# Moving one scatter of the last chunk behind the fetch of the first tile's second rows

## The reference

```python
# 1. linear attention with decay, B=4, H=8, S=768, head_dim 48
y[:, :, t] = einsum('bhd,bhde->bhe', rt, state + (u * kt) outer vt)
state = w * state + kt outer vt
x = y as (3072, 384)
# 2. mixture of experts, top 1 of E=8, F=1024, with a skip
do_compute = x @ w_skip > 0
e_idx, gate_w = argmax and top softmax probability of x @ w_gate
x[i] += gate_w * (relu(x[i] @ w1[e]) @ w2[e])      # rows with do_compute
# 3. dense layer, d_ff 2048
h = x @ w_in;  out = (h * clip(h + 3, 0, 6) / 6) @ w_out
```

## Time and profile before

| | us |
|---|---|
| median of 3 runs | 697.08 (696.63 to 697.37) |
| profiled execution, its own time | 699.52 |
| its span in the profile | 697.7 |
| PE busy | 686.7 (98%) |
| DVE busy | 381.7 (55%) |
| ACT busy | 323.8 (46%) |
| POOL busy | 141.2 (20%) |

### The profile page before, as it was taken

One profiled execution on the slowest core, in us unless ns is written; L12 is line 12 of the kernel. 1 busy time (PEld: TensorE's weight loads), 2 busy tenths in 40 slices (PEclk: granted clock), 3 DMA queues, 4 the chain that ended last, 5 costly groups with the idle time before them and its releaser, 6 DMA issues.

```text
span 697.7 us, 13712 instructions
## 1 busy us (share of the span) xinstructions
PE 686.7 (98%) x5072; PEld 623.7 (89%) x5072; DVE 381.7 (55%) x788; ACT 323.8 (46%) x704; POOL 141.2 (20%) x190
## 2 busy tenths in 40 slices
PE   7999999999999999999999999999999999999998
PEld 5888888879999999899999999999999989998997
DVE  5677667678777777666543443343434333434333
ACT  5777777735555555554433333233333333324222
POOL 8757966543232321100000000000000000000000
PEclk9999999999999999999999999999999999999999
DMA  7888876718666668320023004000500050001001
GB/s 137 186 201 198 186 170 153 238 39 294 232 216 211 223 208 279 104 25 1 1 60 32 1 1 84 7 1 0 92 1 0 1 91 1 0 1 47 0 1 45
DMA packets 135161, 65.70 MB, mean 94 GB/s; under 512 B 110724, under 2 KB 130696, under 8 KB 135104
## 3 DMA queue, kind: packets, MB, share of 16 engines
q1 hardware_dynamic: 131088, 60.13, 33.6%
q0 software_dynamic: 2560, 4.60, 2.1%
q10 hardware_dynamic: 1456, 0.20, 0.2%
HBM read 53.37 MB, written 12.48 MB: 94 GB/s over the span
## 4 chain that ended last, share of the span: by engine, by line
PE 94%; DVE 2%; POOL 1%; issue 1%; DMA 1%; ACT 0%; another core or an unknown queue 0%; DVEq 0%; ACTq 0%; POOLq 0%
PE bank_A L1038 8%; PE bank_A L1039 8%; PE bank_A L1037 8%; PE bank_L L1037 4%; PE bank_L L1039 4%; PE bank_L L1038 4%; PE bank_P L1039 4%; PE bank_P L1038 4%; PE bank_P L1037 4%; PE bank_kT L1038 4%; PE bank_kT L1039 4%; PE bank_kT L1037 4%; PE bank_A L954 4%; PE bank_YT L1039 3%; PE bank_YT L1038 3%; PE bank_YT L979 3%
## 5 line engine op out<-in xcount | busy, mean ns | idle before, releaser
L1595 DVE TENSOR_TENSOR g_lo<-g,g_hi 128x512 fp32r<-128x512 f32 x96 | 66.5, 692 | 67.1 <-ACT g_hi L824 67.1
L824 ACT ACTIVATE g_hi<-g 128x512 fp32r<-128x512 f32 x96 | 60.7, 632 | 73.1 <-DVE g L1593 73.1
L1593 DVE SCALAR_TENSOR_TENSOR g<-cut,bank_A 128x512 f32<-128x512 f32 x60 | 41.2, 687 | 76.4 <-ACT cut L821 76.4
L821 ACT ACTIVATE cut<-bank_A 128x512 f32<-128x512 f32 x60 | 35.8, 597 | 94.2 <-PE bank_A L1039 93.7
L1039 PE MATMUL bank_A<-mT_hi,wi_lo 128*128 128x512 f32 x180 | 71.0, 394 | 0.0
L1038 PE MATMUL bank_A<-mT_lo,wi_hi 128*128 128x512 f32 x180 | 70.9, 394 | 0.0
L1037 PE MATMUL bank_A<-mT_hi,wi_hi 128*128 128x512 f32 x180 | 70.0, 389 | 0.0
L658 ACT ACTIVATE bank_A<-ident,own 128x128 f32<-128x128 f32 x188 | 58.1, 355 | 23.7 <-DVE A_sb L1293 18.7
L1593 DVE SCALAR_TENSOR_TENSOR g<-cut,bank_kT 128x512 f32<-128x512 f32 x36 | 24.7, 687 | 67.5 <-ACT cut L821 67.5
L821 ACT ACTIVATE cut<-bank_kT 128x512 f32<-128x512 f32 x36 | 21.5, 597 | 70.5 <-PE bank_kT L1039 70.5
L1037 PE MATMUL bank_kT<-mT_hi,wi_hi 128*128 128x512 f32 x108 | 42.1, 389 | 0.9 <-DVE mT_lo L1586 0.9
(11 more groups left out here) (333 smaller groups left out, 1807.1 us busy)
## 6 DMA issues: line engine op xcount, KB each, us to landing
raw<-in_moe_w_dram SPq DMA_DIRECT2D x24, 512.0 KB
raw<-in_moe_w_dram SPq DMA_DIRECT2D x7, 1536.0 KB
r_in<-in_r_dram SPq DMA_DIRECT2D x24, 192.0 KB, 3.6
v_in<-in_v_dram SPq DMA_DIRECT2D x24, 192.0 KB, 4.2
x_scratch<-y_sb SPq DMA_DIRECT2D x24, 192.0 KB, 2.3
k_in<-in_k_dram SPq DMA_DIRECT2D x23, 192.0 KB, 3.8
m_in<-x_scratch SPq DMA_DIRECT2D x20, 192.0 KB, 5.5
out_dram<-o_sb SPq DMA_DIRECT2D x10, 384.0 KB, 2.8
```

What stands on the lines that cost most here:

```text
L821: eng.activation(cut[f % 2][:, :], p_H[f % 3][:, :], ACT.Relu, bias=0.5, scale=1.0 / 6.0).then_inc(s_cut, 1)
L824: eng.activation(g_hi[f % 4][:, :], g[f % 2][:, :], ACT.Copy).then_inc(s_ghi, 1)
L1593: eng.scalar_tensor_tensor(g[f % 2][:, :], cut[f % 2][:, :], 1.0, p_H[f % 3][:, :], ALU.min, ALU.mult).then_inc(s_g, 1)
L1595: eng.tensor_tensor(g_lo[f % 4][:, :], g[f % 2][:, :], g_hi[f % 4][:, :].bitcast(F32), ALU.subtract).then_inc(s_glo, 1)
```

## The change

The scatter of b = 1 of the last chunk is taken out of the group in front of the fetch of tile 0's second rows, and put behind that fetch, in front of the scatters of b = 2 and 3. The four scatters keep their order among themselves. The call that issues it repeats its two semaphore waits (`s_id`, `s_slot`).

```diff
             rows_of(0, 0, listed, stored=N - P)
-            scatters(NC - 1, NC - 1, range(0, LATE))
+            scatters(NC - 1, NC - 1, range(0, 1))
             for b in range(B):
                 eng.wait_ge(s_st[b], 16 * NC)
             eng.wait_ge(s_who0, 1)
             rows_of(0, 1, who[0])
+            scatters(NC - 1, NC - 1, range(1, LATE))
             scatters(NC, NC - 1, range(LATE, B))
             n_tiles = tiles_planned(eng)
```

## The result

The changed kernel takes 700.65 us (median of 4 runs, 699.98 to 701.72), the kernel before 697.17 (4 runs, 696.63 to 697.37). The ratio is 1.0051, with a 95% interval of 1.0038 to 1.0064: slower by 0.5%, 3.5 us. My range ended at 699.0.

A forecast was written before the change was run, and what follows sets the result against it. TensorE, 94% of the chain that ended last, was taken as the bound. Tile 0's fetch, the weights and tile 1's first and second rows each cost 0, so the forecast stayed at the median, 697.1 us, range 696.5 to 699.0.

The forecast's parts named there:

- The chain of delays: Scatters behind tile 0's second fetch: one more slot delays table load, POOL's copy and tile 1's fetches by 1.28 us.
- the second rows of tile 1: Tile 1's second fetch, issued at 162.45: lands between 165.6 and 166.6, cost 0, bounds 0 and 2.6 us.
- the second fetch falls behind w2: Rival at tile 1's second fetch: TensorE waits up to 2.6 us, 699.7, or 701.4 with the clock; chance 0.16.
- The slack: TensorE's transposes of tile 1: 1.0 us between landing and use for the first rows, 1.2 us for the second.
- The fetch of the change: Tile 0's second fetch: released by `s_who0`, not the scatter, so taking the scatter away gains 0.
- w1's slip and the first rows: Tile 1: w1 issued 0.2 us later, first rows landing at 165.4 against 166.23; both cost 0.
- my rival with a short wait: Rival at tile 1's transposes: TensorE waits 0.1 to 1.3 us, time 697.2 to 698.4; chance 0.18.
- The price of the clock: TensorE after an idle stretch of 1.2 us: lower clock costs 1.7 us, giving 701.4 in the rival behind w2.
- The queue order: DMA queues at tile 1's fetches: POOL's packets go only when what q1 had queued ahead is gone, not in turn.

The follow-up runs named there:

- e0: The kernel before, unchanged, run again for a second profile: 696.93 us.
- e8: The kernel before with 30 small memsets delaying only tile 1's fetches on POOL, run again for a profile without the pause: 700.09 us, ratio 1.0031.
- e9: The changed kernel again, unaltered, on the first chip: 702.50 us, ratio 1.0075 to the kernel before.
- e10: The kernel before, unchanged, again on the first chip to read its slack: 697.98 us.
- e3: The kernel before with 12 small memsets on POOL ahead of the copy of tile 1's row numbers, delaying only tile 1's fetches: 696.90 us, ratio 1.0000.
- e7: The changed kernel with the scatter of b = 0 also moved behind tile 0's second fetch: 704.21 us, ratio 1.0080 to the kernel before.
- e5: The changed kernel with SP holding tile 1's w2 until POOL has issued both of tile 1's fetches: 698.60 us, ratio 1.0003 to the kernel before.
- e1: The changed kernel with SP holding tile 1's w2 until tile 1's second rows have landed: 699.58 us, ratio 1.0040 to the kernel before.
- e2: The changed kernel with 16 filler transposes between TensorE's transposes of tile 1's first and second rows: 699.90 us, ratio 1.0043 to the kernel before.
- e4: The kernel before with 30 half-size memsets on POOL, delaying only tile 1's fetches: 702.11 us, ratio 1.0048.
- e6: The changed kernel with TensorE's transposes of tile 1's second rows moved behind the next eight products of tile 0: 699.88 us, ratio 1.0022 to the kernel before.

## Why the prediction was wrong

**The chain of delays was right.** One more slot behind the fetch, the table load later, POOL's copy and tile 1's fetches later, TensorE's transposes as the place where it shows: all of it is in the rows. The fetch moved by 1.08 us against e0 (I had 1.28); the chain started 0.31 us earlier.

**The step that failed is the second rows of tile 1**: "I take a landing between 165.6 and 166.6: the fetch comes into the slow beginning of w2, where it meets less than the fetches of 159.67 and 161.17 met. Cost 0." It landed 6.2 us behind its issue where I took 3.2 to 4.2, and in e8 and e9 7.6. That term I put at 0, and it measured a wait of 1.97 us and 1.53 us of low clock behind it. A slow beginning of w2 does not mean that the engines have little queued: in the earlier trace rows the share is 96.9% while little is moved. I read the MB and not the share. My own rival "the second fetch falls behind w2" was nearest to the true case, with 0.16 for its chance. Its size, 2.6 us of wait and 1.7 of clock against 1.97 and 1.53, came out partly by luck: it had all of w2 ahead of the fetch, while the fetch was through with some 630 of w2's 1024 packets moved (by 165.5), and it counted on 1.2 us of slack that was not there. The start from which it counted w2, "about 164.6", follows from no row.

**The slack was read from a single execution.** I took 1.0 and 1.2 us from the profile with the pause, in which the second fetch landed after 4.2 us. In e0 it took 5.6 us and in e10 5.1, so that the second rows' landing and TensorE are level in e0 (163.9 and 163.92) and 0.35 us apart in e10. TensorE's own distance from the fetch's issue hardly differs (5.46, 5.62 and 5.45 us). I had noted that the profiled execution was 2.44 us above the median, and did not ask where those 2.44 us stood. DVE's 2.40 us of idle time before L1375 was in the timeline.

**The fetch of the change was read right for that profile, and not for all.** That the scatter "could have been 2.28 - 0.30 = 1.98 us longer before it touched the fetch" holds with the pause, and with idle times of 1.33 and 1.85 us also in e3 and e10. In e0 and e8 the fetch starts 0.30 us behind the scatter, which did hold it, but not for long: in e0 `s_who0` was raised by 145.66, and 0.93 us behind that is 146.59, against a start at 146.84. So the change can give 0.25 us there; the rest of the 0.54 us between 146.84 and 146.30 is an execution that started earlier. The transposes that use this fetch stand at 150.88 in e0, 4.0 us behind its start, so nothing shows that even the 0.25 us reach TensorE.

**w1's slip and the first rows** cost nothing in the profile after, as predicted; in e9 the first rows cost 0.42 us. The wait of 1.97 us is by itself 0.28% and above the 1.3 us of my rival with a short wait; with the clock behind it, it is 0.5%.

**The price of the clock** was taken from one idle stretch of 1.2 us. It came near, but an idle stretch of that length doesn't always bring the clock down (last section).

**The queue order** was half right: in these windows POOL's packets go behind what was queued before them, and not in turn with it (e7). The Trainium skill's rule of one packet from each queue in turn ("DMA: Bandwidth & Descriptors", section "Queues, rings and completion order") is not what these windows show: 3 packets of q0 beside 454 of q1 in e7, and none beside 125 after. By that rule, as I had it, the fetch would land some 3 us behind its issue, near 162.4 and ahead of TensorE, and the change would have cost nothing. That all of the fetch's packets stood ready in these windows, and that the profile counts the packets that the rule speaks of, isn't shown.

## What to carry to other kernels

When a step on a slow queue is pushed back, look for the next large transfer that another queue issues close behind it, and compare the two issue times: here a lead of 1.6 us over a load of 1.5 MB shrank to 0.2, and 3.5 us were lost; in the profiles without the pause there was no wait at 0.64 (e3), and 1.86 and 3.32 us at 0.19 and 0.17. A wait on the issuing engine that keeps that order (e5) took the loss away, but gained nothing over the kernel before, and held too long (e1) it only moves the loss to the other load. And read a slack of the size of a transfer's scatter from more than one profile: three profiles of the kernel before gave 1.2, 0 and 0.35 us for the same wait.

## What the runs showed of the hardware

- The DMA engines can be busy while little moves: between 1.0 and 2.5 us behind its issue, w2 in the earlier trace rows moved 0.19 MB at a share of 96.9%. Few bytes are thus no sign of a free engine.
- A transfer issued 0.2 us ahead of a load of 1536 KB by another queue landed behind much of it. POOL's first packets come later than SP's: those of the fetch issued at 149.91 in the profile before began at 151.5, 1.6 us behind, and those of w2 issued at 213.46 began at 214.5, 1.0 us behind. An issue time on POOL and one on SP are not the same moment for the engines. By these two, packets come level at a lead of about 0.6 us (an estimate, without the queues ahead), and it is below 0.64 that the table turns.
- In or behind idle stretches of TensorE of 1.86 us (after), 2.96 (e7), 3.14 (e9) and 3.32 (e8) the clock fell to the lower level of 1.2 GHz each time, and with one of 0.74 us behind fillers (e2) it did not. Between them the length alone doesn't tell: near 145 us, 1.21 us (before), 1.37 (e4), 1.39 (e7) and 1.41 (e6) were followed by stretches of 2 us at 0.50 to 0.60, and 1.37 us in e5 by none below 1.00. Nor did the clock fall behind 1.18 us in e1 and 1.19 us in e6, some 25 us later in the kernel. The low clock cost 1.53 us in the changed kernel.
- Both the fetch and w2 have almost no slack. w2 held back by 3.75 us (e1) made TensorE wait 1.18 us in tile 1's first layer, so the fetch can't be protected by delaying w2 at will; e5 held it back until the fetch was issued, and TensorE did not wait.
